# w3 tiles transposed by VectorE in 32x32 blocks, w_out's rows in another order, and the last tile of an attention-and-experts kernel by halves

## The reference

```python
# attention: q, k, v (2, 8, 768, 64), proj (64, 6)
q_bucket = sum((q @ proj > 0) * 2 ** arange(6)); k_bucket likewise
scores = where(q_bucket[:, None] == k_bucket[None, :], q @ k.T / 8, -1e9)
x = softmax(scores) @ v                      # then (1536, 512)
# gated layer: w1, w2 (512, 1024), w3 (1024, 1024), w_out (1024, 512)
x = ((x @ w1) * (x @ w2)) @ w3 @ w_out
# four experts: w1 (4, 512, 1024), w2 (4, 1024, 512)
p = probs / (probs.sum(-1) + 1e-9)
out = sum(p[:, e] * (relu(x @ w1[e]) @ w2[e]) for e in range(4))
```

## Time and profile before

| what | value |
|---|---|
| median of 3 runs | 981.53 us (981.4 to 982.41) |
| the profiled execution's own time | 981.78 us |
| its span | 980.0 us |
| granted TensorE clock | full in all of the span (2.4 GHz) |
| TensorE busy, VectorE, ScalarE, GpSimd | 99%, 60%, 46%, 36% |
| stage 0, attention begins | about 62 us |
| last VectorE instruction to the end | 976.81 to 980.0 us |

### The profile page before, as it was taken

The page is one execution under the profiler, slowest core; times in us unless marked ns, Lnnn a source line. Parts: engine busy times, 40 slices in busy tenths (PEclk is TensorE's granted clock), DMA queues, the critical chain, the costliest instruction groups (busy, mean ns, idle before and its releaser), DMA issues.

```text
span 980.0 us, 15717 instructions
## 1 busy us (share of the span) xinstructions
PE 973.1 (99%) x5385; PEld 904.4 (92%) x5385; DVE 591.2 (60%) x955; ACT 455.3 (46%) x844; POOL 355.9 (36%) x348
## 2 busy tenths in 40 slices
PE   8999999999999999999999999999999999999998
PEld 6889999999999999999998988989889899898997
DVE  4469999999987780678654453443624435354442
ACT  4258888888885552555540331413404134042230
POOL 1113564556764320335171340512505226043130
PEclk9999999999999999999999999999999999999999
DMA  8436877765445330301110201102010020100102
GB/s 256 125 76 159 213 210 200 207 169 135 109 146 159 113 113 1 112 2 44 44 44 1 65 22 43 43 1 66 22 43 27 16 63 22 43 22 21 43 28 101
DMA packets 89869, 81.55 MB, mean 83 GB/s; under 512 B 33376, under 2 KB 72416, under 8 KB 89824
## 3 DMA queue, kind: packets, MB, share of 16 engines
q1 hardware_dynamic: 89824, 80.97, 29.5%
HBM read 54.69 MB, written 7.39 MB: 63 GB/s over the span
## 4 chain that ended last, share of the span: by engine, by line
PE 98%; DVE 1%; DMA 1%; SPq 0%; issue 0%; ACT 0%
PE ps L315 25%; PE ps L316 25%; PE ps L317 25%; PE ps L1521 6%; PE ps L1508 4%; PE ps L1536 3%; PE ps L1538 3%; PE ps L1510 3%; PE ps L1487 1%; PE ps L1469 1%; PE ps L1418 1%; PE ps L1475 1%; PE ps L1478 1%; DMA stage<-in_moe_w_out 1%; DVE expo L1089 0%; DVE pT_lo L1103 0%
## 5 line engine op out<-in xcount | busy, mean ns | idle before, releaser
L702 POOL TENSOR_TENSOR v_sum<-kept,kept 128x384 f32<-128x384 f32 x48 | 49.1, 1022 | 355.3 <-ACT kept L857 355.3
L857 ACT COPY kept<-ps 128x384 f32<-128x384 f32 x144 | 68.5, 478 | 213.8 <-PE ps L317 212.9
L1383 DVE SCALAR_TENSOR_TENSOR acc<-ps,gate,acc 128x512 f32<-128x512 f32 x96 | 72.0, 750 | 140.1 <-PE ps L317 140.1
L317 PE MATMUL ps<-v_hi,hid_lo 128*128 128x512 f32 x384 | 149.6, 390 | 0.0
L316 PE MATMUL ps<-v_lo,hid_hi 128*128 128x512 f32 x384 | 149.5, 389 | 0.0
L315 PE MATMUL ps<-v_hi,hid_hi 128*128 128x512 f32 x384 | 149.4, 389 | 0.0
L1232 DVE TENSOR_TENSOR u_sum<-ps,kept 128x384 f32<-128x384 f32 x48 | 26.8, 557 | 122.7 <-PE ps L317 122.7
L1089 DVE TENSOR_SCALAR_CACHE_REDUCE expo<-ps 128x768 f32<-128x768 f32 x96 | 91.7, 956 | 14.1 <-PE ps L1510 10.6
L788 ACT ACTIVATE expo<-expo,neg_max 128x768 f32<-128x768 f32 x96 | 90.5, 942 | 8.0 <-DVE expo L1089 5.8
L1103 DVE TENSOR_TENSOR pT_lo<-ps,pT_hi 128x768 fp32r<-128x768 f32 x96 | 90.5, 947 | 3.7 <-ACT pT_hi L802 3.4
L802 ACT CAST pT_hi<-ps 128x768 fp32r<-128x768 f32 x96 | 76.6, 798 | 24.8 <-PE ps L1521 24.5
(11 more groups left out here) (164 smaller groups left out, 2368.5 us busy)
## 6 DMA issues: line engine op xcount, KB each, us to landing
w_raw<-gate_sums SPq DMA_DIRECT2D x16, 512.0 KB, 3.6
e_raw<-in_moe_w SPq DMA_DIRECT2D x64, 128.0 KB, 2.3
v_raw<-in_moe_w SPq DMA_DIRECT2D x32, 256.0 KB, 3.3
w_raw<-in_moe_w SPq DMA_DIRECT2D x48, 128.0 KB, 3.5
made_raw<-in_moe_w SPq DMA_DIRECT2D x16, 256.0 KB, 3.6
gate_sums<-made SPq DMA_DIRECT2D x8, 512.0 KB, 2.7
raw_qk<-in_q SPq DMA_DIRECT2D x16, 192.0 KB, 3.0
raw_qk<-in_k SPq DMA_DIRECT2D x16, 192.0 KB, 3.4
```

Source lines behind the costliest of these rows:

```text
L317: return nc.tensor.matmul(out_ps, lhs_lo, rhs_hi, start=False, stop=stop, skip_group_check=onto)
L702: nc.gpsimd.tensor_tensor(v_sum[:, :], kept[s][1][:, :], kept[s][2][:, :], ALU.add).then_inc(v_done, 1)
L857: nc.scalar.copy(kept[s][n][:, :], ps[4 * s + n][:, 0:HALF]).then_inc(kept_done, 1)
L1383: nc.vector.scalar_tensor_tensor(acc[:, t, :], ps[4 * ((h + t // 4) % 2) + t % 4], gate_f[:, bass.ds(t * E + e, 1)], acc[:, t, :], ALU.mul ...
```

## The change

- w3's tiles 3 to 7 are no longer transposed by TensorE. Each is loaded by eight DMAs of 64 KB so that its 32-row groups lie where the blocks belong, and VectorE transposes all its 32x32 blocks in one instruction (turn_w3) into w3T_raw in SBUF, from which ScalarE and VectorE make the high and low part.
- These tiles have four places of their own (w3_more), so tiles 2 to 5 are loaded without a wait; 6 and 7 wait for tile 2's transposes and for tile 3's turn. All their loads come earlier in SP's queue: tile 2 before q and k, tile 3 behind them, tile 4 ahead of v, the rest behind it.
- Column h\*512 + 4n + k of w3 is now entry n of piece (h, k), for the blocks' sake; w_out's rows are loaded in the same order (every fourth row), and the transposes left on TensorE read their columns at a stride of four elements.
- The last token tile of the last round is multiplied, added and stored in two halves of 256 columns, the second in another PSUM bank. On TensorE the last expert is written out instead of being the last turn of the loop.

```diff
+    PE_TILES = 3
+    BLOCK = 32
+    BLOCKS = P // BLOCK
+        w3T_raw = [place(f"w3T_raw{n}", [P, FK, P], F32, wout_at) for n in range(2)]
+        w3_more = [place(f"w3_more{n}", [P, F], F32, fold_at) for n in range(4)]
...
+        wout_tiles = moe_w_out.rearrange("(h p k) n -> h k p n", h=2, p=P)
+        w3_blocks = moe_w3.rearrange("(t b i) (h a c) -> t a i b h c", b=BLOCKS, i=BLOCK, h=2, a=BLOCKS)
+        def w3_place(it):
+            return w3_raw[it] if it < 2 else w3_more[(it - 2) % 4]
+        def tile_parts(last, t):
+            return (slice(0, D // 2), slice(D // 2, D)) if last and t == ALL_TILES - 1 else (slice(0, D),)
+        def down_bank(h, t, n):
+            t -= 4 * n
+            return ps[4 * ((h + t // 4) % 2) + t % 4]
...
-                sp.dma_start(stage[kt][:, :], moe_w_out[kt * P:(kt + 1) * P, :]).then_inc(stage_loaded[kt], 16)
+                sp.dma_start(stage[kt][:, :], wout_tiles[kt // 4, kt % 4, :, :]).then_inc(stage_loaded[kt], 16)
...
-            def load_w3(it, par):
-                sp.wait_ge(w3T_mm, w3T_count(it - 2, 2) if isinstance(it, int) else 2 * (it - 1))
-                sp.dma_start(w3_raw[par][:, :], w3_tiles[it, :, :]).then_inc(w3_loaded[par], 16)
+            def load_w3(it):
+                loaded = w3_loaded[(it - 2) % 4]
+                if it < PE_TILES:
+                    sp.dma_start(w3_place(it)[:, :], w3_tiles[it, :, :]).then_inc(loaded, 16)
+                else:
+                    if it == 6:
+                        sp.wait_ge(w3T_mm, w3T_count(2, 2))
+                    elif it == 7:
+                        sp.wait_ge(w3_turned, 1)
+                    for a in range(BLOCKS):
+                        raw = w3_place(it)[a * BLOCK:(a + 1) * BLOCK, :].rearrange("i (b h c) -> i b h c", b=BLOCKS, h=2)
+                        for h in range(2):
+                            sp.dma_start(raw[:, :, h, :], w3_blocks[it, a, :, :, h, :]).then_inc(loaded, 16)
+            load_w3(2)
             load_qk(0, 0, True)
+            load_w3(3)
...
-            load_w3(2, 0)
-            load_w3(3, 1)
+            load_w3(4)
             load_v(0, 0, True)
             load_qk(0, 1, True)
             load_v(0, 1, True)
-            with sp.Fori(2, FK // 2) as m:
-                for par in range(2):
-                    load_w3(2 * m + par, par)
+            for it in range(5, FK):
+                load_w3(it)
...
+                else:
+                    act.wait_ge(w3_turned, it + 1 - PE_TILES)
+                    act.wait_ge(wp_mm, it - 1)
+                    nc.scalar.copy(w3T_hi[par][:, 4 * lo:4 * hi, :], w3T_raw[par][:, 4 * lo:4 * hi, :])\
+                        .then_inc(w3T_hi_done, hi - lo)
...
+            def turn_w3(it, par):
+                dve.wait_ge(w3_loaded[(it - 2) % 4], 16 * 2 * BLOCKS + (16 if it == 6 else 16 * 2 * BLOCKS if it == 7 else 0))
+                if it >= 2 + PE_TILES:
+                    dve.wait_ge(w3T_lo_done, w3T_count(it - 2, 2))
+                nc.vector.transpose(w3T_raw[par][:, :, :].rearrange("p (h k) (b i) -> p b h k i", h=2, i=BLOCK),
+                                    w3_place(it)[:, :].rearrange("p (b h j k) -> p b h k j", b=BLOCKS, h=2, j=BLOCK))\
+                    .then_inc(w3_turned, 1)
...
             wout_low(7)
+            turn_w3(3, 1)
             for half in halves(2):
                 w3T_low(2, 0, half)
...
                 if it == 2:
                     constants()
+                if it + 2 < FK:
+                    turn_w3(it + 2, it % 2)
...
+                columns = w3_place(it)[:, :].rearrange("p (h n k) -> p h k n", h=2, n=P)
                 for kt in range(4 * lo, 4 * hi):
-                    last = nc.tensor.transpose(ps_w3T[par][:, kt // 4, (kt % 4) * P:(kt % 4 + 1) * P],
-                                               w3_raw[par][:, kt * P:(kt + 1) * P], ident[:, :])
+                    last = nc.tensor.transpose(ps_w3T[it % 2][:, kt // 4, (kt % 4) * P:(kt % 4 + 1) * P],
+                                               columns[:, kt // 4, kt % 4, :], ident[:, :])
...
                 first_prep(2 * it - 2)
                 if it < FK - 1:
-                    transpose_w3(it + 1, (it + 1) % 2, False)
                     first_prep(2 * it - 1)
...
+                        for n, cols in enumerate(tile_parts(last and h == ROUNDS - 1, t)):
+                            if n:
+                                pe.wait_ge(acc_done, ALL_TILES * r + 8)
+                            for p in range(PIECES):
...
+                                done = mult3(down_bank(h, t, n)[:, cols], hid_hi[:, B * p + b, toks],
+                                             hid_lo[:, B * p + b, toks], v2_hi[p][:, cols], v2_lo[p][:, cols],
+                                             p == 0, p == PIECES - 1)
+                            done.then_inc(down_mm, 1)
...
-            with pe.Fori(1, E) as e:
-                expert(e, False)
+            with pe.Fori(1, E - 1) as e:
+                expert(e, False, False)
+            expert(E - 1, False, True)
```

More of the change, by code:

```diff
@@ L243, in build_program @@
         first_w3_loaded = [[sem(f"first_w3_loaded{n}_{h}") for h in range(2)] for n in range(2)]
-        w3_loaded = [sem(f"w3_loaded{n}") for n in range(2)]
+        w3_loaded = [sem(f"w3_loaded{n}") for n in range(4)]
         qk_loaded = [sem(f"qk_loaded{n}") for n in range(2)]
@@ L522, in store @@
             def store(t, tiles):
-                sp.wait_ge(acc_done, ALL_TILES * (E * ROUNDS - 1) + t + tiles)
                 b, tt = t // TILES, t % TILES
-                sp.dma_start(out_tokens[b, :, tt:tt + tiles, :], acc[:, t:t + tiles, :]).then_inc(stored, 16)
+                for n, cols in enumerate(tile_parts(True, t)):
+                    sp.wait_ge(acc_done, ALL_TILES * (E * ROUNDS - 1) + t + n + tiles)
+                    sp.dma_start(out_tokens[b, :, tt:tt + tiles, cols], acc[:, t:t + tiles, cols]).then_inc(stored, 16)
             for g in range(RAWS, GATE_ALL):
@@ L763, in _, with w3T_high @@
         def _(act):
-            def w3T_high(it, par, first, half=(0, 2)):
+            def w3T_high(it, par, half=(0, 2)):
                 lo, hi = half
-                act.wait_ge(w3T_mm, w3T_count(it, hi))
-                if not first:
+                if it < PE_TILES:
+                    act.wait_ge(w3T_mm, w3T_count(it, hi))
+                    if it > 1:
+                        act.wait_ge(wp_mm, it - 1)
+                    nc.scalar.copy(w3T_hi[par][:, 4 * lo:4 * hi, :].rearrange("p (a c) n -> p a (c n)", a=hi - lo),
+                                   ps_w3T[par][:, lo:hi, :]).then_inc(w3T_hi_done, hi - lo)
+                else:
+                    act.wait_ge(w3_turned, it + 1 - PE_TILES)
                     act.wait_ge(wp_mm, it - 1)
-                nc.scalar.copy(w3T_hi[par][:, 4 * lo:4 * hi, :].rearrange("p (a c) n -> p a (c n)", a=hi - lo),
-                               ps_w3T[par][:, lo:hi, :]).then_inc(w3T_hi_done, hi - lo)
+                    nc.scalar.copy(w3T_hi[par][:, 4 * lo:4 * hi, :], w3T_raw[par][:, 4 * lo:4 * hi, :])\
+                        .then_inc(w3T_hi_done, hi - lo)
             def wp_high(it):
@@ L862, in _ @@
             first, second = halves(0)
-            w3T_high(0, 0, True, first)
+            w3T_high(0, 0, first)
             wout_high(0)
-            w3T_high(1, 1, True, first)
+            w3T_high(1, 1, first)
             for j in range(1, 5):
                 wout_high(j)
-            w3T_high(0, 0, True, second)
+            w3T_high(0, 0, second)
             wout_high(5)
-            w3T_high(1, 1, True, second)
+            w3T_high(1, 1, second)
             wout_high(6)
@@ L879, in _ @@
             for half in halves(2):
-                w3T_high(2, 0, False, half)
+                w3T_high(2, 0, half)
             wp_high(0)
@@ L1641, in _ @@
             pe.wait_ge(ident_ready, 1)
-            transpose_w3(0, 0, True, first)
+            transpose_w3(0, first)
             run_on_zeros(2)
-            transpose_w3(1, 1, True, first)
+            transpose_w3(1, first)
             begin_wp(0, 0)
@@ L1649, in _ @@
                 multiply_wp(1, 1, (kt,))
-            transpose_w3(0, 0, True, second)
+            transpose_w3(0, second)
             multiply_wp(0, 0, (3,))
             multiply_wp(1, 1, (3,))
-            transpose_w3(1, 1, True, second)
+            transpose_w3(1, second)
             multiply_wp(0, 0, (4, 5))
@@ L1657, in _ @@
             for half in halves(2):
-                transpose_w3(2, 0, False, half)
+                transpose_w3(2, half)
             multiply_wp(1, 1, (6,))
@@ L1722, in multiply_y, with expert @@
                         part(n, ft, ft == 0, ft == FT_ORDER[-1])
-            def expert(e, first):
+            def expert(e, first, last):
                 for h in range(ROUNDS):
```

36 lines of the change are left out of this document (17 added, 19 removed).

## The result

| | before | after |
|---|---|---|
| median | 981.46 us | **986.12 us** (985.06 to 986.77, six runs) |
| ratio, with its interval | | 1.0045 (1.0033 to 1.0058) |
| the profiled execution | 981.78 us, span 980.0 | 985.06 us, span 983.3 |
| tile 3's multiplication starts (first matmul's record) | 29.74 us | 33.69 us |
| third VectorE pass of attention (expo) | 62.37 us | 66.15 us |

The first two expo passes stand before it in both, at 58.03 and 60.29 us before and at 62.03 and 64.06 after: attention begins there, beside the last tile of w3, and the 62 us of the table of before are the third pass.

The account below looks back on a forecast made before the run. TensorE, working 973.1 of 980.0 us, was taken as the bound. Part 1's 2.0 us and the tail's 0.17 gave 2.2 us off 981.78; less 0.25 for the median, 979.3 us, range 978.2 to 982.3.

Parts of the forecast that it names:

- part 1: Start of the kernel: five w3 tiles leave TensorE, 4.35 us of transposes removed, 2.0 us gained after waits.
- the other arm of the same wait: Head 0's step 2 on TensorE needs GpSimd's q_cross, which follows v's landing: v issued at 21.1 us, q_cross done 28.95.
- 15 issues of 0.44 us: SP's queue: 15 more load issues ahead of v at 0.44 us each, 6.6 us in all.
- rival B: SP's queue makes v late and the kernel slower; at 0.60 us an issue the gain is gone; chance 0.13.
- VectorE free at 29.16 us: VectorE before bits in head 0: constants() ends at 27.86 us, then tile 4's turn takes 1.3 us.
- I expect TensorE idle for about 1.5 us: TensorE would wait about 1.5 us just before head 0's step 3 or step 2, where it is idle nowhere today.
- The turn: 1.3 us: VectorE's transpose of one 128x1024 fp32 tile was taken as 1.3 us, near the 1.22 us of w3T_lo.
- rival A: Strided reads cost double: turn 2.3 us, kernel 980.3 us, or 982.0 if weight loads double too; chance 0.2.
- The gate row: VectorE's gate reads 12 elements at a 16-byte stride in 172 ns, 173 contiguous; taken as evidence that strided reads cost nothing extra.
- Weight loads: zero: Strided column reads in TensorE's transposes of the three remaining tiles: no added time; 1.74 us if the read halves.
- w_out's order: Loading w_out's rows 8 KB apart, still as 2-KB pieces, at the start: no cost.
- The granted clock: A clock below full in the first 40 us, possibly from new idle time, listed as a sign of error without a price.

Follow-up runs that it names:

- e5: The changed kernel with VectorE's transposes reading their input contiguously instead of at a stride of four (another product): 985.92 us, a single run.
- e6: The changed kernel with 19 idle bf16 matmuls on TensorE ahead of steps 2 and 3 of the first heads: 986.02 us.
- e1: The changed kernel with v's first load issued directly behind the first q and k, ahead of w3's tiles 3 and 4: 983.19 us.
- e7: e1 with VectorE's turn of tile 4 moved behind bits: 981.31 us.
- e2: The kernel before with only w_out's rows in the new order and all eight w3 tiles' columns read by TensorE at a stride of four: 983.13 us.
- e3: The kernel before with only w_out's rows loaded in the new order (another product): 983.14 us, a single run.
- e12: e11 with the turn of tile 3 moved behind wp_low(0): 980.99 us.
- e4: The kernel before with only w3's columns read at a stride of four by TensorE's transposes (another product): 982.12 us, a single run.
- e11: e7 with seven instead of two matmuls on zeros at the start and constants() called before VectorE's loop: 980.26 us.
- e9: e2 with seven instead of two matmuls on zeros between the first transposes of w3's tiles 0 and 1: 982.99 us.

## Why the prediction was wrong, step by step

**v's load (part 1, "the other arm of the same wait"): the step that failed.** The forecast had v issued at 21.1 us and q_cross done at 28.95. v was issued at 23.91 and q_cross done at 32.27. The term "15 issues of 0.44 us" was wrong for eight of them: tile 3's took 8.03 us, 8.80 to 16.83, of which 3.43 and 1.70 us in single ones. The other issues ahead of v took 0.43 to 0.60, tile 4's eight 3.75 together; v's own took 1.73, which put its landing 1.3 us later still (in e5 and e6 it took 0.43, and why it was long is not known). Counted over the traces, SP came to stand with some 2,150 packets issued and not done (before at 8.28 us, after at 8.80) and went on when they had drained to some 1,770 (before at 10.5 us, after at 12.2). So the prediction's own rival B was what happened, in mechanism (SP standing "just behind the two q/k loads", with 1,024 pieces more) and in sign; its chance, 0.13, and its form, so many tenths on every issue, were off, and the queue did not fill a second time over tile 4. e1 shows it by moving one issue: 2.9 us of 4.7.

**VectorE free at 29.16 us, measured 32.28: the second step.** With v early (e1) the kernel still takes 983.19 us, slower than before and outside the range, so v's load is not the whole error. The forecast let VectorE end constants() at 27.86 us as before and turn tile 4 in 1.3. In after constants() and the code ahead of it began 1.4 us later, for the start was late, its gate stood 1.25 us behind GpSimd, and the turn took 0.7 more. In e1 it was w3T_lo that stood, for 1.3 us, and VectorE came free at 31.5. e7, which takes the turn out of the way, gives 1.9 us more.

**"I expect TensorE idle for about 1.5 us".** It was 3.3: 1.6, 1.0 and 0.7 us, and the first two not for VectorE. The bits' wait came out at 0.7 us because GpSimd was later still, by the 0.69 us for which VectorE stood idle before bits. The mechanism, bits behind VectorE's order, is nevertheless right: e1 bares it (1.6 us), and e7 removes it for 1.9.

**The turn: 1.3 us, measured 2.01.** Nearer to rival A's 2.3 than to the row. The gate row could not carry it: at e5's rate, 0.77 us for 1024 elements, twelve elements would show 9 ns, and the row compares two different operations under a fixed part of 170 ns. The rule of the Trainium skill that the prediction named against itself ("SBUF — State Buffer", section "Door 1: The DMA port swizzle") was right, and e5 is the trace that agrees. In after it is not on the chain: the turn ended at 32.28 us, and bits had to wait till 32.95 for L1531, which itself waited for q_cross. In e1 it lay on the chain.

**Weight loads: zero, measured 0.09 us a tile.** 211 ns instead of 140, mostly hidden. Right in size for a term of zero; it is also in tile 2's 0.96.

**w_out's order: "nothing", measured 1.2 to 1.5 us.** An unpriced edit on the one stretch in which TensorE waits for its loads at the start. That its pieces have the same size was taken for the same cost. e2 and e3 show it; in after it moved tile 2 and VectorE's constants(), not the end, for the wait on v absorbed it.

**The granted clock: named under "wrong", given no price.** It took 1.5 us in the profiled run. A forecast that expects TensorE idle needs a price for what comes behind the idle time as well.

**What the rest gave.** Tile 5 and 7: 0.87 each, right. Tile 6: 0.30 forecast, 0.08 measured; the wait is 0.57 as taken from the earlier trace rows, but step 1 then takes 0.55 us where the earlier trace rows has 0.33. In the tail the halves pass in 0.12 us as computed, and VectorE's last takes 0.48; 0.43 us less where 0.17 was forecast, since the rest to the end fell from 2.44 to 2.15 us. SP was free of its loads at 39.07 us, not 34; nothing waited for that in after.

**What was not foreseen at all** is that a part read from SBUF makes VectorE wait for GpSimd. In after it hit the gate, q_cross being later still, and head 1's q_cross, which was not yet needed; neither is on the chain. In e1, e5, e6, e7 and e12 it lies on the way to bits or to step 2.

## What to carry to other kernels

When a load is moved behind a block of small ones, count the packets outstanding on the queue at that point, and not only the issues: behind some 2,150 of them a single issue took 3.43 us here instead of 0.44, and what hangs on the load must be counted from there. Put the load with the longest chain behind it first; here that one line was worth 2.9 us and the whole intended saving was 2.2. When an operand moves from PSUM to SBUF, look at which GpSimd instructions run beside its reader.

## What the runs showed of the hardware that was not expected

- SP's issue of one 64-KB DMA lasted 3.43 us. In before, after and e1 alike this first stand ended with some 1,770 packets undone. The second one (1.70 us, in after and e1) ended with only 900 or so, and v's own 1.73 us in after had some 300 in front of it, so no single number of packets is shown to be a limit of the queue, and what ends a stand stays open.
- VectorE instructions that read SBUF alone stood still beside GpSimd's q_cross or v_parts: w3T_lo 2.55 us for 1.22, code 1.92 for 0.28, dp_sum_eps 1.74 for 0.17; in after one of gate's four took the group from 0.42 to 1.67 us. The turn, which also reads SBUF alone, did not: in after it ran beside q_cross from 30.42 us on in its usual 2.01 us. It goes the other way too: in after q_cross took 2.81 us from 49.82 us on, 1.0 us more than its work, for VectorE's w3T_lo had begun at 49.70 and lasted till 50.93. GpSimd in order of time:

```profile
49.82 2.81 POOL L600 TENSOR_TENSOR q_cross<-qk_T,q_main 128x768 fp32r<-128x768 f32 x1 [0.18 <-POOL q_main L597]
```

- The first 256-KB piece of w_out took about 160 to 210 ns a packet with rows 8 KB apart, 92 to 100 with rows in order. Later pieces mostly took 84 to 113 ns either way; single ones reached 151 to 163 in after and e1, and in e4 with the old order, so packets alone there don't separate the two.
- Still open: the spread of the versions with v early (981.64 to 986.6 us in e1, 980.1 to 984.35 in e7, 979.64 to 983.22 in e11; before, 981.22 to 982.41 in six runs and 980.96 to 983.74 in the 27 that stood beside e9 to e11). Their single profiles show late landings of tile 3, low-clock matmuls and waits on moved one-hots, in different mixtures; in e1 the slow half is the half with the granted clock below full. How much each gives was not settled.
